# Top-32 attention with two feed-forward layers on one core: slots 0 to 16 reordered, four staging buffers, q/k scratch in whole rows

## The reference

```python
scores = (q @ k.T) / 8                        # batch 4, heads 8, 576 tokens, 64 dims
kth = np.partition(scores, -32)[..., -32]     # the 32nd largest of each row
scores = np.where(scores >= kth, scores, -1e9)
x = softmax(scores) @ v                       # then to (2304, 512)
h = x @ w_in;  g = h if h >= 1, 0 if h <= -1, else (h + 1)**2 / 4   # 512 -> 2048
y = g @ w_out                                 # 2048 -> 512, first layer
h = max(y @ w2_in, 0);  out = (h * h) @ w2_out                      # second layer
```

## Time and profile before

| | us |
|---|---|
| median of 3 runs | 1286.64 (1285.8 to 1288.35) |
| the profiled execution | 1287.39 |
| its span | 1285.6 |
| PE busy | 1194.8 (93%) |
| VectorE busy | 910.6 (71%) |
| POOL busy | 783.9 (61%) |
| ScalarE busy | 721.8 (56%) |

### The profile page before, as it was taken

How to read it: one execution, slowest core, us unless ns; L and a number is a source line. 1 busy time by engine, 2 the same in 40 slices (tenths; PEclk the granted TensorE clock), 3 DMA queues, 4 the chain that set the end, 5 groups by cost and what they waited for, 6 DMA issues and landing times.

```text
span 1285.6 us, 24517 instructions
## 1 busy us (share of the span) xinstructions
PE 1194.8 (93%) x8760; PEld 1132.5 (88%) x8760; DVE 910.6 (71%) x2039; ACT 721.8 (56%) x1617; POOL 783.9 (61%) x637
## 2 busy tenths in 40 slices
PE   2677888999999999999999999999999999999998
PEld 1566878988888999999999999999989999999997
DVE  5789899989899998989999999989861111111121
ACT  4555566766655476776767654556543565643332
POOL 2999787787788776777766767666562222222222
PEclk9966799999999999999999999999999999999999
DMA  5899748565879972543437851445429500780000
GB/s 194 275 341 349 255 164 274 187 232 209 321 254 341 387 300 74 170 166 122 130 114 263 314 197 39 140 151 198 147 77 354 217 34 1 265 325 8 27 17 17
DMA packets 98728, 245.89 MB, mean 191 GB/s; under 512 B 7344, under 2 KB 48304, under 8 KB 86320
## 3 DMA queue, kind: packets, MB, share of 16 engines
q1 hardware_dynamic: 98608, 244.33, 53.7%
HBM read 167.23 MB, written 77.07 MB: 190 GB/s over the span
## 4 chain that ended last, share of the span: by engine, by line
PE 69%; POOL 11%; ACT 8%; DVE 5%; issue 4%; DMA 1%; SPq 0%; ACTq 0%; POOLq 0%
PE h_ps L581 21%; PE y_ps L602 14%; PE y_ps L596 12%; PE pv_ps L540 6%; PE score_ps L581 6%; POOL s_sb L1045 4%; PE tr_ps L513 4%; POOL prob L1050 3%; PE score_ps L478 3%; DVE top L860 2%; DVE rest L862 2%; ACT prob L699 1%; POOL kq_lo L1029 1%; POOL w_out L1037 1%; ACT s_sb L676 1%
## 5 line engine op out<-in xcount | busy, mean ns | idle before, releaser
L1063 POOL TENSOR_TENSOR g_lo<-g_sb,g_hi 128x256 fp32r<-128x256 f32 x288 | 217.2, 754 | 405.1 <-ACT g_hi L778 404.9
L581 PE MATMUL h_ps<-xt_hi,w_in 128*128 128x256 f32 x1880 | 391.3, 291 | 3.5 <-DVE xt_lo L908 2.0
L581 PEld LDWEIGHTS h_ps<-xt_hi,w_in 128*128 128x128 f32 x1880 | 309.6, 191 | 6.7 <-issue 3.0
L860 DVE MAX8 top<-rest 128x8 f32<-128x576 f32 x432 | 303.8, 744 | 0.0
L1045 POOL TENSOR_SCALAR s_sb<-s_sb,top 128x576 f32<-128x576 f32 x144 | 258.4, 1794 | 51.5 <-DVE top L860 50.6
L581 PE MATMUL h_ps<-xt_lo,w_in 128*128 128x256 f32 x940 | 266.2, 283 | 0.0
L596 PE MATMUL y_ps<-g_hi,w_out 128*128 128x256 f32 x1152 | 232.6, 285 | 0.4 <-POOL g_lo L1063 0.3
L778 ACT ACTIVATE g_hi<-g_sb 128x256 fp32r<-128x256 f32 x288 | 121.0, 420 | 184.7 <-DVE g_sb L917 68.8
L862 DVE MATCH_REPLACE8 rest<-top,rest 128x576 f32<-128x576 f32 x288 | 211.4, 741 | 0.0
L602 PE MATMUL y_ps<-w_out,g_hi 128*128 128x512 f32 x576 | 203.3, 394 | 0.3 <-POOL g_lo L1063 0.3
L596 PEld LDWEIGHTS y_ps<-g_hi,w_out 128*128 128x128 f32 x1152 | 190.4, 193 | 1.7 <-POOL g_lo L1063 0.5
(11 more groups left out here) (79 smaller groups left out, 1954.9 us busy)
## 6 DMA issues: line engine op xcount, KB each, us to landing
w_in<-w_scratch SPq DMA_DIRECT2D x32, 1024.0 KB, 6.7
w_out<-w_scratch SPq DMA_DIRECT2D x32, 1024.0 KB, 8.0
ks<-ks_scratch SPq DMA_DIRECT2D x47, 576.0 KB, 5.5
qs<-qs_scratch SPq DMA_DIRECT2D x78, 256.0 KB, 4.4
stage<-in_w_dram SPq DMA_DIRECT2D x32, 512.0 KB, 4.7
w_scratch<-w_in SPq DMA_DIRECT2D x16, 1024.0 KB, 6.8
w_scratch<-w_out SPq DMA_DIRECT2D x16, 1024.0 KB, 8.3
v_sb<-in_vv_dram SPq DMA_DIRECT2D x48, 325.0 KB, 5.5
```

Source lines behind the costliest of these rows:

```text
L581: last = pe.matmul(h_bank(k), wi[:, f // 2, w, m, cols], x[:, m, :], start=(m == 0 and n == 0), stop=(m == KT - 1 and n == 2))
L860: dve.max(best, src[:, :]).then_inc(rank_step, 1)
L1063: pool.tensor_tensor(g_lo[k % 2][:, :], g_sb[k % 2][:, :], g_hi[k % 2][:, :].bitcast(F32), ALU.subtract).then_inc(g_lo_done, 1)
```

## The change

- The slots of the q/k pieces and of the first layer's blocks are other ones; from slot 0 to 17 no slot but 0, 14 and 15 has more than one such job, and 14 and 15 have a block for POOL and one for VectorE. From slot 19 on two blocks or a block and a piece can still meet.
- The first layer's blocks are staged in four buffers: the two of before and xr and ys, which are not in use until slot 18. The first three are staged before slot 0, the next three in slots 0, 1 and 2, the others one slot ahead of their use.
- POOL makes one kq_lo or weight lo part of the slot before the second step's g_lo instead of after it. This holds for all slots.
- POOL, not VectorE, makes the first kq_lo. The second query tile's half of `split_first` stands behind the first ranking round of VectorE.
- VectorE's three normalising operations stand one round later.
- The scratch of q and k is one tensor of whole rows, three DMAs per piece instead of six; a qs tile comes in two DMAs instead of one. The restack stands first in SP's slot.
- Waits are added that keep the staging buffers from being overwritten and the lo parts' semaphores in order.

```diff
-PREP_SLOT = (-1, 0, 2, 4, 7, 9, 13, 15, 17, 28, 30, 32, 38, 41, 44, 47)
+PREP_SLOT = (-1, 1, 3, 5, 11, 13, 17, 19, 29, 31, 33, 35, 38, 41, 44, 47)
-W1_PER_SLOT = (1, 2, 1, 2, 1, 2, 1, 1, 1, 1, 1, 1, 1)
+W1_SLOT = [-1, 0, 0, 2, 4, 6, 7, 8, 9, 10, 12, 14, 14, 15, 15, 16]
+STAGE_SLOT = [-1, -1, -1, 0, 1, 2] + [s - 1 for s in W_SLOT[6:]]
 def by_vector(i):
-    return i >= WBLOCKS and i % 2 == 1
+    return i in (12, 14) or (i >= WBLOCKS and i % 2 == 1)
+def stage_at(i):
+    return i % 4 if i < WBLOCKS else i % 2
-    ks_dram = [scratch(f"ks_scratch{g}", [2, 2 * DIM, SEQ]) for g in range(PREPS)]
-    qs_dram = [scratch(f"qs_scratch{g}", [QT, 2, 2 * DIM, 2, P]) for g in range(PREPS)]
+    kq_dram = [scratch(f"kq_scratch{g}", [3, 2 * DIM, KQ]) for g in range(PREPS)]
...
             def restack(at):
                 for x, part in enumerate((kq_hi, kq_lo)):
-                    sp.dma_start(ks_dram[g][x, :, :], part[:, 0:SEQ].bitcast(F32)).then_inc(restacked, 16)
-                    for var in range(2):
-                        sp.dma_start(qs_dram[g][:, x if var == 0 else 1 - x, :, var, :]
-                                     .rearrange("t p n -> p t n"),
-                                     part[:, SEQ:KQ].rearrange("p (t n) -> p t n", t=QT)
-                                     .bitcast(F32)).then_inc(restacked, 16)
+                    sp.dma_start(kq_dram[g][x, :, :], part[:, :].bitcast(F32)).then_inc(restacked, 16)
+                sp.dma_start(kq_dram[g][2, :, SEQ:KQ], kq_hi[:, SEQ:KQ].bitcast(F32)).then_inc(restacked, 16)
             def load_qs(g, t, i):
-                sp.dma_start(qs[i][:, :, :, :].bitcast(F32),
-                             qs_dram[g][t].rearrange("x (d h) v n -> (x d) h v n", h=2)).then_inc(qs_loaded[i], 16)
+                cols = slice(SEQ + P * t, SEQ + P * (t + 1))
+                for var in range(2):
+                    sp.dma_start(qs[i][:, :, var, :].bitcast(F32),
+                                 kq_dram[g][var:var + 2, :, cols].rearrange("x (d h) n -> (x d) h n", h=2)
+                                 ).then_inc(qs_loaded[i], 16)
             def stage_block(i):
-                if i >= 2:
+                if i >= WBLOCKS:
                     sp.wait_ge(w_lo_done[i % 2], i // 2)
+                elif i >= 4:
+                    sp.wait_ge(w_lo_done[i % 2], i // 2 - 1)
             def slot(n):                                        # SP
+                if n and n - 1 in PREP_SLOT:
+                    restack(PREP_SLOT.index(n - 1))
 ...
-                if n and n - 1 in PREP_SLOT:
-                    restack(PREP_SLOT.index(n - 1))
             load_first()
             load_kq(0)
             load_v(0, 0, 0)
-            stage_block(0)
+            for i in range(3):
+                stage_block(i)
             restack(0)
-            load_kq(1)
...
-            split_first(0)                                      # ScalarE
-            split_first(1)
+            split_first(0, 0)
+            split_first(1, 0)
             copy_scores(0, 0)
+            split_first(0, 1)
             copy_scores(0, 1)
-            split_kq(0)
+            split_first(1, 1)
+            split_new(-1)
...
                 both(0)                                         # VectorE
+                if n == 0:
+                    split_first(0, 1)
+                    split_first(1, 1)
-                if past:
-                    add_to_total(n - 2)
                 both(1)
                 at(3 * n)
                 if past:
-                    invert_total(n - 2)
+                    add_to_total(n - 2)
                 both(2)
                 if past:
+                    invert_total(n - 2)
+                both(3)
+                if past:
                     scale_pv(n - 2)
-                both(3)
                 at(3 * n + 1)
...
                 lo_at(q)                                        # POOL
-                lo_at(q + 1)
                 if n in PREP_SLOT:
                     split_kq(PREP_SLOT.index(n))
-                for i in range(2 * WBLOCKS):
-                    if W_SLOT[i] == n:
-                        split_w(i)
+                for i in new_blocks(n)[:1]:
+                    split_w(i)
+                lo_at(q + 1)
+                for i in new_blocks(n)[1:]:
+                    split_w(i)
...
+            split_kq(0)                                         # POOL, ahead of slot 0
+            for i in new_blocks(-1):
+                split_w(i)
```

More of the change, by code:

```diff
@@ L125, in by_vector, with staged_count @@
 def by_vector(i):
-    return i >= WBLOCKS and i % 2 == 1
+    return i in (12, 14) or (i >= WBLOCKS and i % 2 == 1)
+def stage_at(i):
+    return i % 4 if i < WBLOCKS else i % 2
+def staged_count(i):
+    return i // 4 + 1 if i < WBLOCKS else WBLOCKS // 4 + (i - WBLOCKS) // 2 + 1
 def own_bank(k):
@@ L221, in build @@
         zeroed = sem("zeroed")
-        w_staged = [sem(f"w_staged{i}") for i in range(2)]
+        w_staged = [sem(f"w_staged{i}") for i in range(4)]
         first_loaded = [sem(f"first_loaded{i}") for i in range(2)]
@@ L404, in load_x @@
                 sp.wait_ge(x_lo_done, 2 * j)
+                sp.wait_ge(w_lo_done[0], WBLOCKS // 2)
                 layer, c = JOBS[j]
@@ L646, in _, with split_first @@
         def _(act):
-            def split_first(t):
+            def split_first(t, a):
                 act.wait_ge(first_loaded[t], 16)
-                act.activation(ks[0][:, t, :], first_k(t), ACT.Copy).then_inc(first_hi, 1)
-                for a in range(2):
-                    for var in range(2):
-                        rows = slice(DIM * var, DIM * (var + 1))
-                        act.activation(qs[a][rows, t, var, :], first_q(t, a)[rows, :],
-                                       ACT.Copy).then_inc(first_hi, 1)
+                if a == 0:
+                    act.activation(ks[0][:, t, :], first_k(t), ACT.Copy).then_inc(first_hi, 1)
+                for var in range(2):
+                    rows = slice(DIM * var, DIM * (var + 1))
+                    act.activation(qs[a][rows, t, var, :], first_q(t, a)[rows, :],
+                                   ACT.Copy).then_inc(first_hi, 1)
             def split_kq(g):
@@ L939, in clear_corners, with split_first @@
                         dve.memset(prob[n % 2][rows, col:col + TAIL], 0.0).then_inc(zeroed, 1)
-            def split_kq(g):
-                dve.wait_ge(kq_hi_done, g + 1)
-                dve.tensor_tensor(kq_lo[:, :], kq_lo[:, :].bitcast(F32), kq_hi[:, :].bitcast(F32),
-                                  ALU.subtract).then_inc(kq_lo_done, 1)
-            def split_first(t):
-                dve.wait_ge(first_hi, 5 * t + 1)
-                low = slice(DIM, P)
-                dve.tensor_tensor(ks[0][low, t, :], first_k(t)[low, :], ks[0][low, t, :].bitcast(F32),
-                                  ALU.subtract).then_inc(first_lo, 1)
-                for a in range(2):
-                    dve.wait_ge(first_hi, 5 * t + 3 + 2 * a)
-                    for var in range(2):
-                        rows = slice(DIM * var, DIM * (var + 1))
-                        dve.tensor_tensor(qs[a][rows, t, 1 - var, :], first_q(t, a)[rows, :],
-                                          qs[a][rows, t, var, :].bitcast(F32),
-                                          ALU.subtract).then_inc(first_lo, 1)
+            def split_first(t, a):
+                if a == 0:
+                    dve.wait_ge(first_hi, 3 * t + 1)
+                    low = slice(DIM, P)
+                    dve.tensor_tensor(ks[0][low, t, :], first_k(t)[low, :], ks[0][low, t, :].bitcast(F32),
+                                      ALU.subtract).then_inc(first_lo, 1)
+                dve.wait_ge(first_hi, 3 * t + 3 if a == 0 else 8 + 2 * t)
+                for var in range(2):
+                    rows = slice(DIM * var, DIM * (var + 1))
+                    dve.tensor_tensor(qs[a][rows, t, 1 - var, :], first_q(t, a)[rows, :],
+                                      qs[a][rows, t, var, :].bitcast(F32),
+                                      ALU.subtract).then_inc(first_lo, 1)
             def split_w(i):
@@ L1064, in lo_at, with new_blocks @@
                                        ALU.subtract).then_inc(g_lo_done, 1)
+            def new_blocks(n):
+                return [i for i in range(2 * WBLOCKS) if W_SLOT[i] == n and not by_vector(i)]
             def slot(n):
```

42 lines of the change are left out of this document (23 added, 19 removed).

## The result

The changed kernel takes 1298.86 us (median of 4 runs, 1297.16 to 1299.41); the kernel before, run beside it, 1287.49 (4 runs, 1285.8 to 1289.47). The ratio is 1.0084, interval 1.0068 to 1.01: slower by 0.84%, where 1% faster was forecast. The profiled execution took 1297.16 us for a span of 1295.4, so 9.8 us of span have to be found.

A forecast was written before the change was run, and what follows sets the result against it. PE was taken as the bound from 398.7 us, POOL from 52.9 to 129.5, waits before. Terms -7.5 - 4.2 + 2 - 1.5 - 1.5 = -12.7 took 1287.39 to 1274.7, median 1274.3; 8-in-10 range 1265 to 1283.

The forecast's parts named there:

- Start, -7.5: Slots 0 to 2: earlier first scores and fewer waits start slot 3 at 45.4 instead of 52.9; bounds -10 and -4.
- Slots 3 to 9, -4.2: Slots 3 to 9: one POOL job per slot gives 10.15 us each, 72.4 instead of 76.6; bounds -6 and +2.
- rival (b): Small gain: slots 3 to 9 stay near 11 us, bound by half-clock PE and the DMA queue; 1281 us, chance 0.17.
- Slots 10 to 17, +2: Slots 10 to 17: -2 from POOL's reordering, +4 from two weight blocks each in slots 14 and 15; bounds -1 and +5.
- putting the job ahead of that g_lo fills the wait: I give 0.5 us in each of four slots: Slots 12 to 17: POOL's split goes before the second step's g_lo, filling its 2.09 us wait for g_hi; -2 us.
- the pairs in slots 14 and 15: Slots 14 and 15: two weight blocks each, one by VectorE, cost 2 us per slot, +4 in all.
- Slots 18 to 28, -1.5: Slots 18 to 28: slot 19 +1, slot 28 -0.5, less overlap of POOL's and VectorE's blocks -2; bounds -4 and +2.
- no longer on top of: Slots 18 to 28: POOL's block some 3 us before VectorE's, whose subtraction falls from 1.69 to 1.21; -2 us taken.
- Slot 19 gets kq beside a weight block: +1: Slot 19: a kq piece meets a weight block there, costing 1 us.
- Restack and loads, nothing beyond 1 us: Reload stretch: restack 6 to 7 us, ks landing 7 later, two us of slack; nothing booked beyond 1 us.
- slots 29 to 71, -1.5: Slots 29 to the end: PE full; POOL's earlier kq removes some PE waits for a masked prob; bounds -2.5 and 0.
- Rival (a): Slower: ks lands late where restack and load take over 2 us more than counted, PE stands; about 1295 us, chance 0.09.

The follow-up runs named there:

- both_undone: The changed kernel with POOL's old order and the four late q/k pieces split one slot earlier (28, 30, 32, 34): 1283.62 us, ratio 0.9973 to the kernel before.
- old_pool_order: The changed kernel with POOL's new order alone undone (second step's g_lo first, then the split): 1290.89 us, ratio 1.0038 to the kernel before.
- before_new_order: The kernel before with POOL's new order alone (split ahead of the second step's g_lo): 1298.61 us, ratio 1.0096.
- the table of four: Four kernels, late pieces at 28 to 34, against the kernel before: g_sb early, POOL's old order -3.0 us, new +7.5; g_sb later, old -9.3, new -21.0.
- spread_jobs: The changed kernel with POOL's old order, late pieces at 28 to 34, one job per slot where possible, first-layer blocks all POOL's: 1278.68 us, ratio 0.9933.
- kq_one_slot_earlier: The changed kernel with only the four late q/k pieces split one slot earlier (28, 30, 32, 34): 1294.1 us, ratio 1.0051 to the kernel before.
- P and K: Theories on the changed kernel: POOL's new order puts its split beside VectorE's g_sb; the late pieces' kq load is too late. Both undone: 1283.62 us.
- the kq move: The four late q/k pieces split in slots 28, 30, 32, 34 instead of 29, 31, 33, 35; alone in the changed kernel 1294.1 us.
- the late g_sb: The changed kernel with VectorE's second-step g_sb behind the next ranking pair: 1280.08 us; with the late pieces at 28 to 34 as well, 1266.61.

## Why the prediction was wrong

- **Start, -7.5**: -9.1, right. Slot 1 begins at 20.64 (20.9 forecast) and takes 9.64, the floor; slot 3 begins at 43.83 (45.4), inside the bounds. How near it came is partly luck: both_undone and old_pool_order, the same up to slot 27, have slot 3 at 41.5 and 46.1. The wait for pv in slot 2, 4.06 before, was forecast as 3.1:
```profile
36.62 0.16 DVE L888 TENSOR_SCALAR total<-pv_ps 128x2 f32<-128x2 f32 x1 [2.61 <-PE pv_ps L557]
```
- **Slots 3 to 9, -4.2**: -5.2, right. Slots of 9.97 us with POOL idle ahead of the masks, but for slot 6 at 11.33 and slot 8 at 10.22. The floor is VectorE's; TensorE, busy 56 of 71.4 us at a granted clock of 0.65, was not in the way, so rival (b) is out.
- **Slots 10 to 17, +2**: +10.0. The step that failed is "putting the job ahead of that g_lo fills the wait: I give 0.5 us in each of four slots". It does fill POOL's wait, but the same rows 7 have VectorE's g_sb 1.5 us ahead of that g_lo, with two SBUF inputs, in the very time in which the split was put. In place of -2 the order costs +7.2 in this stretch of the changed kernel and +4.8 in that of the kernel before; over the whole span it costs the kernel before 12 us (before_new_order) and the changed one 6 to 10.5 (old_pool_order, the table of four). That the pairs in slots 14 and 15 cost 2 each held (2.6 and 1.7 between both_undone and spread_jobs; 14.75 and 14.77 us for 13.5 to 14.5 in the changed kernel, the collision among it).
- **Slots 18 to 28, -1.5**: +3.4. POOL's block "no longer on top of" VectorE's came true: seven of VectorE's eight subtractions took 1.20 us there, where seven took 1.63 to 1.69 before. But the block came to lie on g_sb instead, and the new order gained nothing up to slot 27 against the old (kq_one_slot_earlier and both_undone). The other miss is "Slot 19 gets kq beside a weight block: +1". In both_undone, with the old order, slots 19, 20 and 21 take 2.3, 1.7 and 1.3 us more than before; with the piece in slot 18 (spread_jobs) slot 19 is back at 12.59 and the stretch 2.3 us shorter. How the +3.4 divides between the two was not tried by itself.
- **Restack and loads, nothing beyond 1 us; slots 29 to 71, -1.5**: +9.8 in slots 29 to 36. The sum counted restack, ks and q up to TensorE's use. It left out the first transfer of the piece, kq's own load, issued one slot before its split as before, but now in slots 28, 30, 32 and 34, where it took 9.3 to 10.5 us. The restack took 10.2 to 10.5 us in three of them, where 6 to 7 were counted, and the ks load 4.2 to 4.5 for 7. Rival (a) had the kind (a transfer that is late behind a backlog) and nearly the time (1295), but not the place: ks was never late.
- **Whole rows, no term**: -2.6 us in the kernel before.
- Of the sum: from the changed kernel to the forecast's 1274.3 it is 24.6 us. Undoing P and K gives 15.2 of them (1283.6), spreading the pairs of jobs 4.9 more (1278.7). The last 4.4 were not found.

Not settled: what makes the kq move worth 13.5 us under the late g_sb, some 7 with POOL's old order and 4 to 5 in the changed kernel. That slot 31 comes 20 us earlier, into the same backlog of reloads, is my explanation of the first; it was argued, not tried, and it doesn't explain the second, where slot 31 begins at 411.0. The move of the normalising operations behind the second ranking pair was never undone alone.

## What to carry to other kernels

Before moving work of POOL into a gap, look at what VectorE does in that gap: if it is an operation with two SBUF inputs that comes after POOL's has begun, expect it to last until POOL's has ended, as it did here 21 times of 21. If the move is wanted all the same, put a one-input batch of VectorE ahead of that operation, so that the wait for the producer is filled and the collision is all there is; here that turned +7.5 into -21.0 us against the kernel before. And for a piece of work that is moved close to its use, work out every transfer of its chain, the first load included, with the landing times of the stretch in which it will stand.

## What the runs showed of the hardware

A VectorE operation of 128x256 with two SBUF inputs takes 0.43 us alone and up to 2.8 us beside a POOL subtraction of 128x1216. When it begins while that subtraction, or one of 128x1024, runs, it ends 0.28 us after POOL's, in 21 cases of 21 in the changed kernel, and POOL's keeps its length (2.79 in slot 13, 2.80 in the earlier trace rows). Beside the one-input half of POOL's mask (L1063) 79 of them took 0.41 to 0.78 us and most ended before it did. VectorE's ranking operations, with one input, keep their 0.73 to 0.76 us beside a split. At the start of the changed kernel:
```profile
12.28 2.79 POOL L1047 TENSOR_TENSOR kq_lo<-kq_lo,kq_hi 128x1216 fp32r<-128x1216 f32 x1 [10.83 <-ACT kq_hi L678]
12.37 0.75 DVE L882 MATCH_REPLACE8 rest<-top,s_sb 128x576 f32<-128x576 f32 x1
```
The two weight splits side by side of the earlier trace rows show the same thing from both sides. Slot 20 of the kernel before:
```profile
267.37 0.74 POOL L1063 TENSOR_TENSOR g_lo<-g_sb,g_hi 128x256 fp32r<-128x256 f32 x1 [2.36 <-ACT g_hi L778]
267.50 1.69 DVE L965 TENSOR_TENSOR w_in<-stage,w_in 128x1024 fp32r<-128x1024 f32 x1
268.06 3.38 POOL L1037 TENSOR_TENSOR w_out<-stage,w_out 128x1024 fp32r<-128x1024 f32 x1
```
VectorE's began while POOL's g_lo ran and took 1.69 us for 1.21; POOL's next one began while VectorE's ran and took 3.38 for 2.38. In these rows the operation that begins second is the one that stands, on either engine.

A kq load of 608 KB takes 5.6 us from its issue in slot 1 and 9.3 to 10.5 when issued in slots 28 to 34; the DMA share is 0.89 in slots 31 to 36. The landing time to count with is that of the stretch.
